# Feeding the feed-forward stage early: the first chunk's load waits for fewer scatters, and the last weight split moves into the last pair's second job

## The chip, the cores and the metric

The program runs on one core of a Trainium2 chip. The metric is the device time of one execution in microseconds. Engines are named as in the profile: PE (TensorE matmul), PEld (its weight load), DVE (VectorE), ACT (ScalarE), POOL (GpSimd) and SP (SyncE, which here only issues DMAs).

## The reference

Three layers run one behind the other over 4 x 576 = 2304 tokens of width 512, in float32.

```python
# attention: 4 batches, 8 heads, head_dim 64, causal window 128, slope bias, softmax
x = attn_out.transpose(0, 2, 1, 3).reshape(B * S, H * D)            # 2304 x 512
# mixture of experts, 8 experts of 512 -> 1024 -> 512
do_compute = x @ w_skip > 0;  xc = x[do_compute]
logits = xc @ w_gate;  e_idx = argmax(logits);  gate_w = softmax(logits)[e_idx]
for e in range(8):
    h = maximum(xc[e_idx == e] @ w1[e], 0)
    y[e_idx == e] = gate_w * (h @ w2[e])
x[do_compute] = xc + y
# feed-forward 512 -> 2048 -> 512
h = x @ w_in
g = h * tanh(log1p(exp(h)))
out = g @ w_out
```

With the inputs given, 1015 of the 2304 tokens go to an expert. Their counts by expert are 102, 111, 174, 146, 175, 133, 94, 80. Among the first 448 tokens they are 14, 17, 35, 24, 22, 45, 13, 9.

## The kernel before, in words

**Three stages in one program.** `attention` writes x to a DRAM tensor `tokens`, with the gate logits on the side. `experts` sorts the tokens by expert on the chip and corrects their rows in `tokens`. `feed_forward` reads `tokens` chunk by chunk and writes `out`. Every engine runs its own instruction stream, and counters (semaphores) are the only order between them.

**Experts.** Two experts form a pair (p = 0 to 3), and a job is 64 tokens of each of the two, 128 rows. The number of jobs of a pair is counted on the chip, at L984 to L1001, from the counts by expert. It goes to `jobs_i` in SBUF, from where each engine loads it into a register (`jobs_of`, L743). With the counts above, the pairs have 2, 3, 3 and 2 jobs. `all_jobs` (L757) writes job 0 without a condition and the others inside an `If` each: four in a row, then a loop. A job on PE (L1134) is `hidden` twice (32 matmuls), `transpose_h` twice, `output` twice (32 matmuls). DVE does two `relu` and one `scale_y` (L1030), which adds the scaled result to the gathered rows in `y_sb`. POOL gathers the rows of later jobs with an indirect DMA, and scatters `y_sb` to `tokens` (L835); each scatter adds 16 to `y_scattered[p]` when it has landed.

**Weights of the feed-forward stage.** Each fp32 weight is held as a high and a low part (fp32r), and a product takes three matmuls: lo x hi, hi x lo, hi x hi. `w_ffn` is 16 pieces of 1024 columns. Pieces 0 to 13 (`EARLY` = 14) are loaded during attention. ACT makes their high parts (`high_parts`, L902): 0 to 6 ahead of the last pair, 7 to 13 in its job 0. DVE makes the low parts (`low_parts`, L1022): 0 to 5 and 6 and 7 in job 0 of the last pair, 8 to 13 behind its last job (L1057). Pieces 14 and 15 land where the gathered rows `x_in` lie, so they are loaded after the experts, and are split in eight minis of 256 columns during chunk 0 (`SPLIT`, L1186). PE needs the early parts at the first `output`, and the minis at hidden block 12's `output` (L1432).

**Feed-forward.** Six chunks of 384 tokens. The x of a chunk is transposed by PE, and split by ACT (`xt_hi`) and DVE (`xt_lo`). A chunk has 16 steps f. In step f PE runs `hidden(f)`, 12 matmuls of 384 columns, and then `output(f - 3)`, 9 matmuls of 512 columns. Between the two, ACT and DVE work out g of block f: min, exp, a product, ln, exp, products, then `g_hi` and `g_lo`. In steps 3, 6, 9 and 12 (`AHEAD`) PE also transposes a quarter of the next chunk's x. SP issues, in this order: once all scatters of the last pair have landed, three loads of 128 tokens each for chunk 0 (L1278), the two last weight pieces (L1280), then the load of chunk 1 (L1266).

PE ends the experts with 20 dummy matmuls (`keep_warm`, L1156), then waits for the three loads and transposes them tile by tile (L1458).

## Time and profile before

| | |
|---|---|
| Median of 3 runs | 766.01 us (764.3 to 769.79) |
| Profiled execution, its own time | 767.03 us |
| Span in the profile | 765.2 us, mean granted clock 0.991 |
| PE busy | 742.9 us, 97% |
| DVE, ACT, POOL busy | 508.9, 366.6, 107.4 us |
| Experts' last matmul ends | 331.02 us |
| First matmul of the feed-forward proper | 343.97 us |

The span is the profile's own clock, from the first to the last instruction, and the execution's own time is 1.8 us longer. Attention fills the first 150 us, the experts 150 to 331 us, the feed-forward the rest. "Idle before" an instruction names who released it; "issue" there means that the profile shows no releaser. In a table by windows, the column PEclk is TensorE's granted clock, where 1.00 is 2.4 GHz and 0.50 is 1.2 GHz.

### The profile page before, as it was taken

How to read it: one execution, taken by the hardware profiler on the slowest of the kernel's cores; microseconds unless marked ns; L12 is line 12 of the kernel's file. 1: busy time of each engine (PE TensorE's matmuls, PEld its weight loads, DVE VectorE, ACT ScalarE, POOL GpSimd, SP SyncE). 2: the span in 40 equal slices, each digit the busy share in tenths (PEclk: the TensorE clock that was granted, in tenths of full speed). 3: DMA queues.
4: the chain of work that ended last, by engine and by line, in shares of the span. 5: the costliest groups of instructions: out<-in, count | busy, mean ns of one | idle time of the engine just before them, and what ended most of it. 6: DMA issues, size and time to landing. Idle time of an engine off the chain costs nothing.

```text
span 765.2 us, 13541 instructions
## 1 busy us (share of the span) xinstructions
PE 742.9 (97%) x4492; PEld 567.5 (74%) x4492; DVE 508.9 (67%) x1278; ACT 366.6 (48%) x887; POOL 107.4 (14%) x250
## 2 busy tenths in 40 slices
PE   7999999989999999989999999999999999999998
PEld 4887878773333333358989898998988989898986
DVE  4777777641111111647998888888788888888885
ACT  6888888301010103514655554555465545455544
POOL 4656655111110110000000000000000000000000
PEclk9999999989999999999999999999999999999999
DMA  8889988218782660031010101100110101001001
GB/s 300 250 261 279 277 265 234 65 39 327 281 310 87 257 248 23 15 104 41 1 43 1 42 0 42 38 5 2 42 41 0 41 0 41 0 0 42 1 0 42
DMA packets 53244, 78.23 MB, mean 102 GB/s; under 512 B 24739, under 2 KB 26403, under 8 KB 53152
## 3 DMA queue, kind: packets, MB, share of 16 engines
q1 hardware_dynamic: 51136, 72.02, 28.7%
q0 software_dynamic: 1600, 4.85, 1.7%
q8 instruction: 40, 0.66, 0.4%
q10 hardware_dynamic: 432, 0.41, 0.2%
q14 instruction: 36, 0.29, 0.1%
HBM read 65.53 MB, written 12.56 MB: 102 GB/s over the span
## 4 chain that ended last, share of the span: by engine, by line
PE 89%; DVE 5%; issue 2%; DMA 2%; ACT 1%; ACTq 0%; SPq 0%; DVEq 0%; POOLq 0%; POOL 0%
PE ps_y L1438 16%; PE ps_xt L1421 13%; PE ps_ht L1421 12%; PE ps_y L1128 9%; PE ps_h L1110 9%; PE ps_h L1438 8%; PE ps_out_t L586 5%; PE ps_probs_t L569 4%; PE ps_scores L558 4%; PE ps_x L597 4%; DVE h_sb L1020 1%; PE ps_ht L1117 1%; PE ps_h L1407 1%; PE ps_y L88 1%; DMA k_raw<-in_kT 1%
## 5 line engine op out<-in xcount | busy, mean ns | idle before, releaser
L1310 ACT ACTIVATE u_sb<-u_sb 128x384 f32<-128x384 f32 x96 | 50.6, 527 | 107.1 <-DVE u_sb L1358 107.1
L1314 ACT ACTIVATE r_sb<-n_sb,all_consts 128x384 f32<-128x384 f32 x96 | 59.3, 617 | 85.3 <-DVE n_sb L1374 85.3
L390 ACT ACTIVATE probs<-probs,neg_max 128x256 f32<-128x256 f32 (+2 forms) x160 | 72.6, 455 | 14.2 <-DVE neg_max L450 13.9
L1438 PE MATMUL ps_y<-ffn_lo,g_hi 128*128 128x512 f32 x192 | 76.6, 399 | 0.0
L1438 PE MATMUL ps_y<-ffn_hi,g_lo 128*128 128x512 f32 x192 | 75.9, 395 | 0.0
L1438 PE MATMUL ps_y<-ffn_hi,g_hi 128*128 128x512 f32 x192 | 75.7, 395 | 0.0
L1421 PE MATMUL ps_xt<-xt_hi,ffn_lo 128*128 128x384 f32 x192 | 66.9, 348 | 0.8 <-DVE xt_lo L1349 0.8
L1386 DVE SCALAR_TENSOR_TENSOR u_sb<-n_sb,r_sb 128x384 f32<-128x384 f32 x96 | 53.7, 559 | 19.1 <-ACT r_sb L1316 19.1
L1421 PE MATMUL ps_ht<-xt_hi,ffn_lo 128*128 128x384 f32 x192 | 66.0, 344 | 0.0
L1421 PE MATMUL ps_xt<-xt_hi,ffn_hi 128*128 128x384 f32 x192 | 65.5, 341 | 0.0
L1421 PE MATMUL ps_xt<-xt_lo,ffn_hi 128*128 128x384 f32 x192 | 65.4, 341 | 0.0
L1421 PE MATMUL ps_ht<-xt_hi,ffn_hi 128*128 128x384 f32 x192 | 64.9, 338 | 0.0
L1421 PE MATMUL ps_ht<-xt_lo,ffn_hi 128*128 128x384 f32 x192 | 64.8, 338 | 0.0
L1040 DVE SCALAR_TENSOR_TENSOR y_sb<-ps_y,x_in 128x512 f32<-128x512 f32 x10 | 7.5, 751 | 77.0 <-PE ps_y L1128 77.0
L450 DVE CUSTOM_DVE_ANT_0 probs<-ps_scores,bias_sb 128x256 f32<-128x256 f32 (+2 forms) x160 | 49.8, 362 | 8.8 <-PE ps_scores L558 8.6
L1363 DVE TENSOR_TENSOR g_lo<-n_sb,g_hi 128x384 fp32r<-128x384 f32 x96 | 52.6, 548 | 2.6 <-ACT g_hi L1329 2.6
L1020 DVE TENSOR_SCALAR h_sb<-ps_h 128x512 f32<-128x512 f32 x20 | 13.8, 691 | 60.6 <-PE ps_h L1110 60.6
L1374 DVE SCALAR_TENSOR_TENSOR n_sb<-u_sb 128x384 f32<-128x384 f32 x96 | 52.8, 550 | 0.7 <-ACT u_sb L1310 0.6
L1379 DVE TENSOR_TENSOR n_sb<-n_sb,r_sb 128x384 f32<-128x384 f32 x96 | 52.8, 550 | 0.0
L1368 DVE SCALAR_TENSOR_TENSOR r_sb<-u_sb,r_sb 128x384 f32<-128x384 f32 x96 | 52.8, 550 | 0.0
L1316 ACT ACTIVATE r_sb<-r_sb 128x384 f32<-128x384 f32 x96 | 50.4, 525 | 3.0
L919 ACT ACTIVATE h_t<-ps_ht 128x512 f32<-128x512 f32 x10 | 6.0, 598 | 93.5 <-PE ps_ht L1117 93.5
(174 smaller groups left out, 1628.4 us busy)
## 6 DMA issues: line engine op xcount, KB each, us to landing
w_sb<-in_w SPq DMA_DIRECT2D x8, 2048.0 KB, 11.9
ffn_raw<-in_w_ffn SPq DMA_DIRECT2D x16, 512.0 KB, 5.1
experts_even<-in_w SPq DMA_DIRECT2D x16, 512.0 KB, 5.8
experts_even<-in_w SPq DMA_DIRECT2D x4, 2048.0 KB, 12.7
q_raw<-in_qT SPq DMA_DIRECT2D x15, 288.0 KB, 4.1
k_raw<-in_kT SPq DMA_DIRECT2D x15, 288.0 KB, 4.9
v_sb<-in_v SPq DMA_DIRECT2D x16, 256.0 KB, 2.6
tokens<-x_out SPq DMA_DIRECT2D x64, 64.0 KB, 3.9
```

What stands on the lines that cost most here:

```text
L390: nc.scalar.activation(probs[0:n, r, h, 0:w], probs[0:n, r, h, 0:w], ACT.Exp, bias=neg_max[0:n, r, h:h + 1], scale=-1.0, accum_out=sums[0: ...
L1110: m = t_.matmul(ps_h[c][mine, :], x[:, k, mine], weights(p, 0, side, k * F1 + c * half), start=(k == 0), stop=(k == KD - 1))
L1128: m = t_.matmul(ps_y[slot][mine, :], (h_t, h_t2)[c][:, k, mine], weights(p, 1, side, (KD * c + k) * D), start=(c == 0 and k == 0), stop=(c ...
L1310: nc.scalar.activation(u_sb[:, t.r], u_sb[:, t.r], ACT.Exp).then_inc(u_ready, 1)
L1314: nc.scalar.activation(r_sb[:, t.r], n_sb[:, t.f % NB], ACT.Ln, bias=cst["two"]).then_inc(ln_ready, 1)
L1363: v.tensor_tensor(g_lo[:, t2.r], n_sb[:, t2.f % NB], g_hi[:, t2.r].bitcast(F32), ALU.subtract).then_inc(g_lo_ready, 1)
L1368: v.scalar_tensor_tensor(out=r, in0=u, scalar=2.0, in1=r, op0=ALU.subtract, op1=ALU.mult).then_inc(b_ready, 1)
L1374: v.scalar_tensor_tensor(out=n_sb[:, t.f % NB], in0=u_sb[:, t.r], scalar=2.0, in1=u_sb[:, t.r], op0=ALU.add, op1=ALU.mult).then_inc(n_read ...
L1379: v.tensor_tensor(n, n, r, ALU.mult).then_inc(ratio_ready, 1)
L1386: v.scalar_tensor_tensor(out=u, in0=n, scalar=2.0, in1=r, op0=ALU.add, op1=ALU.mult).then_inc(a_ready, 1)
L1421: m = nc.tensor.matmul(ps_h[t.f % HB][:, 0:C], ffn[a][:, at:at + P], b[:, t.par, k], start=(n == 0), stop=(n == 3 * KD - 1))
L1438: m = nc.tensor.matmul(ps_o[i][:, :], a[:, t.r, P * i:P * i + P], ffn[b][:, at:at + D], start=(t.f == 0 and n == 0), stop=(t.f == FT - 1 a ...
```

## The change

The first chunk's load waits for only those scatters of the last pair that can hold its tokens. The job count is taken a second time over the first 4 tiles (448 tokens, the chunk has 384), from the same running counts, with one matmul that takes both columns. `jobs_i` now holds 4 early counts, 4 counts of all, and 3 first-job numbers. The last pair has at least two jobs (`SURE` = 2, an empty one where there are fewer), written without a condition. The three tiles go to buffers that are free by then (`x_first` and two slots of `x_in`). PE transposes them quarter by quarter, and the 20 dummy matmuls are gone. DVE's low parts 8 to 13 move ahead of `scale_y` in job 1 of the last pair. SP issues the last two weight pieces once `scale_y` of the last job and PE's transposes are done, and chunk 1's load behind them once all scatters have landed. The minis move to steps 4, 5, 7, 8, 10, 11 and 13 (two of them). The PSUM banks of the feed-forward are dealt out anew, and PE gets a wait on the last `scale_y`, against a count loaded into a register, ahead of the first `output`.

```diff
-    ps_count = ps_h[0][:, 0:E]
+    ps_count = ps_h[0][:, 0:2 * E]
...
+    def early_jobs_of(eng, p):
+        return eng.value_load(jobs_i[0:1, p:p + 1], min_val=1, max_val=PHASE)
...
-    def all_jobs(eng, total, one):
+    def all_jobs(eng, total, one, sure=1):
...
-        one(0, 0)
-        rest(1)
+        for i in range(sure):
+            one(i, i % 2)
+        rest(sure)
...
-        then(v.tensor_scalar(jobs, jobs, 1.0, None, ALU.max))
+        then(v.tensor_tensor(early_and_all, early_and_all, cst["least"], ALU.max))
...
-            split = p == PH - 1 and isinstance(i, int) and i == 0
+            split = p == PH - 1 and isinstance(i, int) and i < SURE
             relu(p, i, 0)
             relu(p, i, 1)
             if split:
-                low_parts(range(0, 6))
+                low_parts(range(8, EARLY) if i else range(0, 6))
             scale_y(p, i, slot, before)
-            if split:
+            if split and not i:
                 low_parts(range(6, 8))
...
-        low_parts(range(8, EARLY))
...
-        t_.matmul(ps_count, ones, upto_tile[:, TT - 1], start=True, stop=True)
+        t_.matmul(ps_count, ones, upto_tile[:, EARLY_TILES - 1:TT:TT - EARLY_TILES], start=True, stop=True)
...
-        keep_warm(nc, ps_h[0], cst, 20)
...
-    SPLIT = {f: n for n, f in enumerate((1, 2, 4, 5, 7, 8, 10, 11))}
+    SPLIT = {4: (0,), 5: (1,), 7: (2,), 8: (3,), 10: (4,), 11: (5,), 13: (6, 7)}
...
-    ps_h, ps_xt, ps_o = banks[0:HB], banks[HB], banks[HB + 1:]
+    ps_h, ps_xt, ps_o = banks[2:HB] + banks[0:2], banks[HB], banks[HB + 1:]
-    first_xt = ps_o + [ps_xt]
+    first_xt = [ps_xt, ps_o[0]] + ps_h[2:HB]
+    x_early = own["x_early"]
...
-        sp.wait_ge(own["y_scattered"], own["jobs_of"](sp, PH - 1) * 16)
+        sp.wait_ge(own["y_scattered"], own["early_jobs_of"](sp, PH - 1) * 16)
         settled(sp, cst)
         for i in range(CT):
-            sp.dma_start(x_sb[:, i], dram["x"][P * i:P * i + P]).then_inc(tile_loaded[i], 16)
+            sp.dma_start(x_early[i], dram["x"][P * i:P * i + P]).then_inc(tile_loaded[i], 16)
+        total = own["jobs_of"](sp, PH - 1)
+        sp.wait_ge(own["y_scaled"], total)
+        settled(sp, cst)
+        sp.wait_ge(xt_ready, KD)
         for n in range(EARLY, PAIRS):
             sp.dma_start(ffn["raw"][:, n * 1024:n * 1024 + 1024], dram["w_ffn"][n]).then_inc(cst["w_loaded"], 16)
-        sp.wait_ge(xt_ready, KD)
+        sp.wait_ge(own["y_scattered"], total * 16)
+        settled(sp, cst)
         load(1)
...
             if isinstance(t.s, int) and t.s == 0:
                 pe.wait_ge(cst["w_lo_ready"], EARLY)
+                pe.wait_ge(own["y_scaled"], own["jobs_of"](pe, PH - 1))
...
         for i in range(CT):
             pe.wait_ge(tile_loaded[i], 16)
-            for k in range(KD):
-                m = nc.tensor.transpose(first_xt[k][:, P * i:P * i + P], x_sb[:, i, P * k:P * k + P], ident)
-                if i == CT - 1:
-                    m.then_inc(xt_ready, 1)
+        for k in range(KD):
+            for i in range(CT):
+                m = nc.tensor.transpose(first_xt[k][:, P * i:P * i + P], x_early[i][:, P * k:P * k + P], ident)
+            m.then_inc(xt_ready, 1)
```

How the instructions now stand, at three places. PE from the branch behind the last pair's jobs to the first matmul of the feed-forward (L88 is `keep_warm`, L1458 the transposes, L1421 `hidden`); before:

```order
L761 UNCONDITIONAL_BRANCH
L88 MATMUL ps_h<-all_consts 128x216 x20
L1400 UNCONDITIONAL_BRANCH
L1458 MATMUL ps_h<-all_consts,x_sb 128x128
L1458 MATMUL ps_y<-all_consts,x_sb 128x128 x2
L1458 MATMUL ps_h<-all_consts,x_sb 128x128 x2
...
L1421 MATMUL ps_xt<-xt_hi,ffn_lo 128x384
```

With the change (L1477 the transposes, L1438 `hidden`):

```order
L768 UNCONDITIONAL_BRANCH
L1477 MATMUL ps_h<-all_consts,x_first 128x128
L1477 MATMUL ps_h<-all_consts,x_in 128x128 x2
...
L1477 MATMUL ps_xt<-all_consts,x_first 128x128
L1477 MATMUL ps_xt<-all_consts,x_in 128x128 x2
...
L1438 MATMUL ps_ht<-xt_hi,ffn_lo 128x384
```

The dummy matmuls and a branch are gone, and the transposes come in groups of three, one group for each quarter of the width.

PE around the first `output` (L1456), behind `hidden(3)`, with the change; the register load and what belongs to it are new there:

```order
L1438 MATMUL ps_xt<-xt_hi,ffn_hi 128x384
L748 TENSOR_LOAD jobs_i
L748 ISA x2
L1456 MATMUL ps_h<-ffn_hi,g_lo 128x512
L1456 MATMUL ps_h<-ffn_lo,g_hi 128x512
```

The load stands behind the waits for `g_hi` and `g_lo` of block 0, so it begins when these are met.

DVE in the last pair, jobs 0 and 1 (`relu`, low parts, `scale_y`); before, and with the change:

```order
L1020 TENSOR_SCALAR h_sb<-ps_h 128x512 x2
L1027 TENSOR_TENSOR ffn_lo<-ffn_raw,ffn_hi 128x1024 x6
L1035 REGISTER_ALU
L1040 SCALAR_TENSOR_TENSOR y_sb<-ps_y,x_in 128x512
L1027 TENSOR_TENSOR ffn_lo<-ffn_raw,ffn_hi 128x1024 x2
L761 COMPARE_AND_BRANCH
L1020 TENSOR_SCALAR h_sb<-ps_h 128x512 x2
L1040 SCALAR_TENSOR_TENSOR y_sb<-ps_y,x_in 128x512
```

```order
L1029 TENSOR_SCALAR h_sb<-ps_h 128x512 x2
L1036 TENSOR_TENSOR ffn_lo<-ffn_raw,ffn_hi 128x1024 x6
L1044 REGISTER_ALU
L1049 SCALAR_TENSOR_TENSOR y_sb<-ps_y,x_in 128x512
L1036 TENSOR_TENSOR ffn_lo<-ffn_raw,ffn_hi 128x1024 x2
L1029 TENSOR_SCALAR h_sb<-ps_h 128x512 x2
L1036 TENSOR_TENSOR ffn_lo<-ffn_raw,ffn_hi 128x1024 x6
L1049 SCALAR_TENSOR_TENSOR y_sb<-ps_y,x_in 128x512
```

The branch between the two jobs is gone, and six low parts stand ahead of the second `scale_y`.

## Rows read from the trace of the kernel before

**Rows 1.** The page: busy time by engine, and the chain's shares by engine.

```profile
PE 742.9 (97%) x4492; PEld 567.5 (74%) x4492; DVE 508.9 (67%) x1278; ACT 366.6 (48%) x887; POOL 107.4 (14%) x250
...
PE 89%; DVE 5%; issue 2%; DMA 2%; ACT 1%; ACTq 0%; SPq 0%; DVEq 0%; POOLq 0%; POOL 0%
```

**Rows 2.** The chain that ended last, 324 to 409 us: start, length, what.

```profile
323.97 7.04 PE ps_y L1128 x32
...
331.04 0.76 DVE y_sb L1040
...
332.68 4.35 DMA tokens<-y_sb,scatter_list
...
337.99 4.44 DMA x_sb<-tokens
...
342.47 0.34 PE ps_h L1458
...
343.97 3.92 PE ps_xt L1421 x12
...
355.88 0.94 PE ps_h L1438 x3
...
406.02 2.12 PE ps_ht L1421 x12
408.14 0.70 PE ps_h L1438 x3
```

**Rows 3.** Timeline of POOL: start, length, instruction, idle before and releaser.

```profile
317.44 1.09 POOL L835 DMA_INDIRECT tokens<-y_sb,scatter_list  x1 [13.21 <-DVE y_sb L1040]
321.46 0.18 POOL L827 COPY scatter_list<-job_entry 128x1 int32<-128x1 int32 x1 [2.94 <-DMA tokens<-y_sb,scatter_list]
```

**Rows 4.** DMA issues, 300 to 366 us: KB each, median us to landing.

```profile
ffn_raw<-in_w_ffn SPq DMA_DIRECT2D x2, 512.0 KB, 5.7
x_sb<-tokens SPq DMA_DIRECT2D x1, 768.0 KB, 4.5
```

**Rows 5.** Timeline of DVE, the last pair's second job, and low parts behind it.

```profile
322.57 0.69 DVE L1020 TENSOR_SCALAR h_sb<-ps_h 128x512 f32<-128x512 f32 x1 [2.74 <-PE ps_h L1110]
...
331.71 6.89 DVE L1027 TENSOR_TENSOR ffn_lo<-ffn_raw,ffn_hi 128x1024 fp32r<-128x1024 f32 x6
```

**Rows 6.** Timeline of ACT, high parts 7 to 13.

```profile
312.60 6.72 ACT L905 ACTIVATE ffn_hi<-ffn_raw 128x1024 fp32r<-128x1024 f32 x7
```

**Rows 7.** Timeline of PE: the first tiles' transposes, and idle times before later matmuls.

```profile
342.47 0.33 PE L1458 MATMUL ps_h<-all_consts,x_sb 128*128 128x128 f32 x1 [1.31 <-DMA x_sb<-tokens]
342.64 0.38 PE L1458 MATMUL ps_y<-all_consts,x_sb 128*128 128x128 f32 x2
...
355.88 0.47 PE L1438 MATMUL ps_h<-ffn_hi,g_lo 128*128 128x512 f32 x1 [1.65 <-issue]
```

**Rows 8.** Windows: length, busy time of PE, PEld, DVE, ACT, POOL, PEclk, DMA.

```profile
160.00:162.00 2.00, 2.00 (x11) 2.00 (x11) 2.00 (x7) 0.00 (x0) 0.00 (x0) 0.50 0.00 0
...
346.00:347.00 1.00, 1.00 (x4) 1.00 (x4) 0.00 (x0) 0.00 (x0) 0.00 (x0) 0.50 1.02 395
```

**Rows 9.** Timeline of PE, PE idle times at 159 and 203 us.

```profile
159.18 4.27 PE L1074 MATMUL ps_h<-what,at_row 128*128 128x40 f32 x20 [2.32 <-DVE at_row L1011]
...
203.54 1.94 PE L1110 MATMUL ps_h<-w_sb,x_first 128*64 128x512 f32 x8 [1.24 <-issue]
```

**Rows 10.** Timelines of SP and of POOL, 171 to 175 us.

```profile
171.01 15.36 SPq L782 DMA_DIRECT2D w_sb<-in_w  x4
...
174.80 0.18 POOL L811 COPY job_entry<-table 128x1 int32 x1 [6.57 <-issue]
```

**Rows 11.** Timeline of DVE, chunk 0, last instruction of step 14.

```profile
407.15 0.56 DVE L1386 SCALAR_TENSOR_TENSOR u_sb<-n_sb,r_sb 128x384 f32<-128x384 f32 x1 [0.19 <-ACT r_sb L1316]
```

**Rows 12.** Timeline of DVE: a mini, and a wait for issue.

```profile
358.43 0.42 DVE L1393 TENSOR_TENSOR ffn_lo<-ffn_raw,ffn_hi 128x256 fp32r<-128x256 f32 x1
...
552.63 0.56 DVE L1358 TENSOR_SCALAR u_sb<-ps_xt 128x384 f32<-128x384 f32 x1 [2.83 <-issue]
```

More of the change, by code:

```diff
@@ L57 @@
 JOBS = PHASE + PH
+SURE = 2
+EARLY_TILES = 4
 LOG_W = W.bit_length() - 1
@@ L678, in experts @@
     by_pair = scratch(PH * PH).rearrange("p (a b) -> p a b", a=PH)
-    chunks = scratch(E).rearrange("p (a b) -> p a b", a=PH)
-    jobs, ends, first1 = (scratch(PH) for _ in range(3))
+    chunks = scratch(2 * E).rearrange("p (a b) -> p a b", a=2 * PH)
+    early_and_all, ends, first1 = scratch(2 * PH), scratch(PH), scratch(PH)
+    jobs = early_and_all[:, PH:2 * PH]
     tables = ffn["tables"]
@@ L684, in experts @@
     assert used[0] <= SCRATCH, used[0]
-    count_i = sb("count_i", [P, E], I32)
-    jobs_i = sb("jobs_i", [1, 2 * PH], I32)
+    count_i = sb("count_i", [P, 2 * E], I32)
+    jobs_i = sb("jobs_i", [1, 3 * PH], I32)
     table = sb("table", [P, JOBS + PHASE + 12], I32)
@@ L936, in _ @@
                 high_parts(range(7))
-            all_jobs(act, totals[p], functools.partial(one, p, total=totals[p], split=(p == PH - 1)))
+            all_jobs(act, totals[p], functools.partial(one, p, total=totals[p], split=(p == PH - 1)),
+                     SURE if p == PH - 1 else 1)
     @block.vector
@@ L987, in _ @@
         v.tensor_copy(rank_i, rank)
-        then(v.tensor_copy(chunks, count_i[:].rearrange("p (a b) -> p a b", a=PH)))
+        then(v.tensor_copy(chunks, count_i[:].rearrange("p (a b) -> p a b", a=2 * PH)))
         v.tensor_scalar(row_i, rank_i, W - 1, None, ALU.bitwise_and)
         v.tensor_scalar(chunk_i, rank_i, LOG_W, None, ALU.logical_shift_right)
-        then(v.tensor_reduce(jobs, chunks, AX_X, ALU.max))
+        then(v.tensor_reduce(early_and_all, chunks, AX_X, ALU.max))
         v.tensor_copy(row, row_i)
         v.tensor_copy(rank, chunk_i)
-        then(v.tensor_scalar(jobs, jobs, 1.0, None, ALU.max))
+        then(v.tensor_tensor(early_and_all, early_and_all, cst["least"], ALU.max))
         v.tensor_tensor(row, row, side, ALU.add)
@@ L998, in _ @@
         then(v.tensor_reduce(ends, by_pair, AX_X, ALU.add))
-        v.tensor_copy(jobs_i[:, 0:PH], jobs[0:1, :])
+        v.tensor_copy(jobs_i[:, 0:2 * PH], early_and_all[0:1, :])
         then(v.scalar_tensor_tensor(out=first1, in0=ends, scalar=1.0, in1=jobs, op0=ALU.add, op1=ALU.subtract))
-        v.tensor_scalar(jobs_i[:, PH:2 * PH], first1[0:1, :], -1.0, None, ALU.add).then_inc(jobs_ready, 1)
+        v.tensor_scalar(jobs_i[:, 2 * PH:3 * PH], first1[0:1, :], -1.0, None, ALU.add).then_inc(jobs_ready, 1)
         then(v.tensor_tensor(work.rearrange("p t (a b) -> p t a b", a=PH), by_expert.rearrange("p (a b t) -> p t a b", a=PH, b=2),
@@ L1055, in _ @@
         for p in range(PH):
-            all_jobs(dve, totals[p], functools.partial(one, p, before=totals[p - 1] if p else None))
-        low_parts(range(8, EARLY))
+            all_jobs(dve, totals[p], functools.partial(one, p, before=totals[p - 1] if p else None),
+                     SURE if p == PH - 1 else 1)
     @block.tensor
@@ L1332, in step @@
                 xt_part(*ahead, AHEAD[f])
-            if isinstance(c, int) and c == 0 and f in SPLIT:
-                piece = mini(SPLIT[f])
+            for n in SPLIT.get(f, ()) if isinstance(c, int) and c == 0 else ():
+                piece = mini(n)
                 act.wait_ge(cst["w_loaded"], 16 * PAIRS)
@@ L1389, in step @@
                 xt_part(*ahead, AHEAD[f - 1])
-            if isinstance(c, int) and c == 0 and f - 1 in SPLIT:
-                piece = mini(SPLIT[f - 1])
-                dve.wait_ge(cst["w_hi_ready"], EARLY + SPLIT[f - 1] + 1)
+            for n in SPLIT.get(f - 1, ()) if isinstance(c, int) and c == 0 else ():
+                piece = mini(n)
+                dve.wait_ge(cst["w_hi_ready"], EARLY + n + 1)
                 v.tensor_tensor(ffn["lo"][:, piece], ffn["raw"][:, piece], ffn["hi"][:, piece].bitcast(F32),
@@ L1456, in _ @@
             pe.wait_ge(tile_loaded[i], 16)
-            for k in range(KD):
-                m = nc.tensor.transpose(first_xt[k][:, P * i:P * i + P], x_sb[:, i, P * k:P * k + P], ident)
-                if i == CT - 1:
-                    m.then_inc(xt_ready, 1)
+        for k in range(KD):
+            for i in range(CT):
+                m = nc.tensor.transpose(first_xt[k][:, P * i:P * i + P], x_early[i][:, P * k:P * k + P], ident)
+            m.then_inc(xt_ready, 1)
         run_steps(pe, step, LAG)
-CONSTS = {"ident": P, "two": 1, "index_m8": E, "odd": E, "upto": PH * PH, "job1": JOBS, "token": TT, "empty": 1}
+CONSTS = {"ident": P, "two": 1, "index_m8": E, "odd": E, "upto": PH * PH, "job1": JOBS, "token": TT, "empty": 1,
+          "least": 2 * PH}
 TABLES = {"not_before": P, "ones": P, "rows": P, "same_expert": E * TT}
@@ L1524, in shape_constants @@
         "two": np.full((P, 1), 2.0),
+        "least": np.tile([1.0] * (2 * PH - 1) + [SURE], (P, 1)),
     }
```

10 lines of the change are left out of this document (7 added, 3 removed).

## The prediction

> **What bounds the kernel now.** I read the page first: PE is busy for 742.9 of 765.2 us and holds 89% of the chain that ended last [rows 1]. So only time in which PE stands still, does dummy work or runs at the lower clock can be won. The chain of waits around the change says where that is. The last matmul of the experts ends at 323.97 + 7.04 = 331.01 us, and the first of the feed-forward starts at 343.97 us [rows 2]. In those 12.96 us the chain goes through `scale_y` on DVE, the last scatter (it lands at 332.68 + 4.35 = 337.03), the load of x (337.99 + 4.44 = 342.43), a transpose and two splits [rows 2]. PE's 20 dummy matmuls in there do nothing for the result. Then the first hidden block takes 3.92 us, where the same twelve matmuls later take 2.12 [rows 2]; the table by windows gives the reason, a granted clock of 0.50, which is 1.2 GHz, against 1.00 at other times [rows 8]. Last, the first `output` starts at 355.88, 7.99 us after the first hidden block is done (343.97 + 3.92 = 347.89): that is the fill of the DVE and ACT pipeline [rows 2]. PE has run ahead by then and idles 1.65 us before it [rows 7]. From there on the chain is PE alone, so whatever moves the first `output` moves the end.
>
> **Part by part.** All the times below are on the profile's clock.
>
> *The early load.* With the routing of these inputs the first 448 tokens give the last pair 13 and 9 tokens, one job; the early count is 1 of 2. Job 0's scatter, issued at 317.44, has landed when POOL copies its next list at 321.46 [rows 3]. Before, it took 342.43 - 337.03 = 5.40 us from a landed scatter to landed tiles [rows 2]; so now they land by 321.46 + 5.40 = 326.9, 4.1 us ahead of the end of the last job. The load is hidden, and so is the last scatter. If that cover went, each us beyond 4.1 would cost one.
>
> *PE from the last job to the first hidden block.* Transposes can start at 331.01. Before, 1.50 us passed from the last tile's first transpose (342.47 [rows 7]) to the first matmul at 343.97 [rows 2]. Now a quarter is whole after three transposes, not after one; consecutive ones start 0.17 us apart [rows 7], so 2 x 0.17 = 0.34 is added. The first matmul starts at 331.01 + 1.50 + 0.34 = 332.85. That is **11.12 us earlier**. `scale_y` stands ahead of the first `xt_lo` on DVE, but runs from 331.04 for 0.76 us [rows 2], so until 331.80, and the first `xt_lo` has only to be done by 332.85. It costs nothing.
>
> *The clock.* PE no longer has 5 us of mostly idle time ahead of hidden block 0. It should run at 2.4 GHz, in 2.12 us to the next block's start, and with the last matmul's tail (a 128x384 matmul's record is longer than its pitch by about 0.17) in 2.29 to its result, instead of 3.92: **1.63 us**. Result at 335.14.
>
> *Low parts 8 to 13.* Six take 6.89 us [rows 5]. They start when the second `relu` ends, 322.57 + 0.69 = 323.26, and end at 330.15; `scale_y` is not due before 331.04. Their high parts are done at 312.60 + 6.72 = 319.32 [rows 6]. Cost nothing, with 0.9 us of cover; each us beyond it delays `scale_y` and then `xt_lo`.
>
> *The register load.* The wait for the last `scale_y` is met long before. But its count is loaded into a register, behind the waits for `g_hi` and `g_lo`, with PE idle. The trace has no such load on PE in the open. The nearest rows: POOL signals before 171.01, where SP's DMAs start on that signal, and then loads six such registers before its copy at 174.80 [rows 10]. That is 3.79 / 6 = 0.63 us each at most, and in other places they are hidden (0). I take 0.63, since nothing runs beside it here. Bounds 0 and 1.3 (twice, if PE's is slower). **+0.63**. The Trainium skill speaks of about 600 ns as the floor of a tensor load (DMA: Bandwidth & Descriptors, Latency and other measured facts), and elsewhere of about 200 ns a register (Runtime: NRT & Kernel Launch, Instruction fetch mechanics); by the second the sum would be 0.4 us better.
>
> *The first output.* 335.14 + 7.99 + 0.63 = 343.76, against 355.88: 12.12 us earlier.
>
> *The minis.* Weights 14 and 15 are issued at about 333, 5.4 us earlier than before, and take 5.7 us to land [rows 4]; the first mini is at step 4, after 343.8. DVE gets two at step 14, and PE needs them for block 12's `output` in step 15. Before, the last DVE instruction of step 14 ends at 407.15 + 0.56 = 407.71 [rows 11] and that `output` starts at 408.14 [rows 2]. Two minis of 0.42 [rows 12] end by 408.55 at most, 0.4 late; instructions on DVE overlap a little, so I take **+0.3**. Bounds 0 (DVE ahead, since steps 2 and 3 lose their minis) and 0.8.
>
> *Chunk 1's load.* It moves behind the two weight pieces and the last scatter. In the worst case the scatter waits until both pieces have landed, at 333.0 + 0.9 + 5.7 = 339.6; then 0.4 to issue and 4.5 to land [rows 4] makes 344.5. PE's transposes for it come behind the first `output`, nine matmuls at 0.70 / 3 each [rows 2], so at 343.76 + 2.1 = 345.9. Hidden, by 1.4 us at the worst.
>
> *Router and SP.* Twice as many columns in six instructions of 0.2 us, and one register load more on SP, which waits anyway: nothing.
>
> *Sum.* -11.12 - 1.63 + 0.63 + 0.3 = **-11.82 us**. Against the profiled execution's own 767.03 us that makes 755.2. It lies 1.0 us above the median of 766.01, so against the median I forecast **754.2 us**. With a free register load and free minis the sum would be -12.75, or 753.3.
>
> **Rivals.**
>
> *A. The clock falls before the first output.* PE's hole there grows: hidden block 3 ends at 332.85 + 4 x 2.12 + 0.17 = 341.5, and the output starts at 343.76, so 2.26 us of idle, against 1.65 [rows 7]. For it: an idle time of 2.32 us at 159.18 [rows 9] was followed by a granted clock of 0.50 [rows 8]. Against it: the 1.65 us were not, and PE is busy without a break for 8 us ahead. Price: the stretch at 1.2 GHz that began at 344 us cost the 1.63 us worked out above. The one at 160 us may have been longer: a mean clock of 0.991 leaves room for 2 x 0.009 x 765 = 14 us at 1.2 GHz in all. I take once to twice 1.63. Time 755.8 to 757.5.
>
> *B. A taken branch is no longer covered.* The first instructions behind the last pair come by a branch over two jobs and a loop. After the first pair, also of two jobs, PE stood still for 1.24 us at such a branch [rows 9], with no engine to wait for; DVE once for 2.83 [rows 12]. Against it: at this very place PE went on into the dummy matmuls without a hole, and there is one branch fewer. Price 1.2 to 2.8 less DVE's and ACT's slack of 0.4: 755.2 to 757. The Trainium skill says that a taken branch to a target outside the two fetched pages stalls the engine until it is fetched (Runtime: NRT & Kernel Launch, Instruction fetch mechanics); the row at 203.54 agrees, and the one at 331 does not, so the rule alone decides nothing here.
>
> *C. The change does not do what it says.* If the early count came out as 2, the tiles would land near 342.4 as before, at best 1.5 us sooner for want of the weights beside them, PE would idle for 10 us and start at 1.2 GHz, and the register load and the minis add 0.9: 765.5 to 767. Against it is the count of 13 and 9.
>
> *D. Slower.* The clock falls in the hole as in A, and stays at 1.2 GHz, since PE then waits step by step on nothing that would raise it. Every us of PE's full-clock work costs one more, so from 11.8 us of such work, a stretch of 24 us at the lower clock, the kernel is slower than before; through the 13 steps left of chunk 0 (4.2 us each) it would be 754 + 55 = 809. Against it: all such stretches in this trace together have at most 14 us.
>
> **How the numbers follow.** The forecast case 0.62 (its own range 752.5 to 755.5), A 0.17, B 0.12, C 0.03, D 0.02, and 0.04 for something unseen, half of it between -1% and +1%. A difference of 1%, 7.7 us, is about what a measurement here can tell from none; 766.01 less that is 758.35. The forecast, A and B lie below it, C above. Faster 0.93, same 0.05, slower 0.02. For the range the lower end is the sum without register load and minis (753.3) and 1.7 us for how far a median of this kernel may move (runs shown lie 1.7 below and 3.8 above it); the upper end takes in A and B, and 0.7 of that: 751.6 to 758.2.
>
> **What would show it.** Right: PE's first transposes of the feed-forward follow the last job's matmul within 0.3 us and no wait for a DMA; twelve matmuls of hidden block 0 in 2.1 us at clock 1.00; six low parts between `relu` and the second `scale_y`, with DVE still waiting for PE; the first `output` 0.6 us later after `g_lo` than before; PE idle about 0.3 us ahead of step 15's output. Wrong: a granted clock of 0.50 behind the first output (A), idle ahead of the transposes with "issue" (B), tiles landing behind 331 (C), or PE waiting for chunk 1's load in step 3.

## The result, and the profile after

The changed kernel takes 756.17 us (median of 4 runs, 753.83 to 757.14) against 767.04 us for the kernel before on the same chip (4 runs, 764.3 to 769.79). The medians are 10.9 us apart. The ratio, which is estimated from all these runs and is not the quotient of the medians (0.9858), is 0.9842, with a 95% interval of 0.9816 to 0.9869: 12.1 us less, between 10.0 and 14.1. The forecast was 754.2 us (751.6 to 758.2). The profiled execution took 753.83 us by its own time, with a span of 752.0 us at a mean granted clock of 0.991, the clock of the profile before.

The page of the changed kernel, where [rows 1] stood before, says that the bound is the same: PE lost 9.5 us of work (40 matmuls fewer: each of the 20 dummies shows as two) and 3.7 us of idle time, and the DMA's share of the chain is 1% instead of 2%, by the page's rounding.

```profile
PE 733.4 (98%) x4452; PEld 559.9 (74%) x4452; DVE 509.6 (68%) x1278; ACT 366.7 (49%) x887; POOL 107.2 (14%) x250
...
PE 89%; DVE 5%; issue 2%; ACT 2%; DMA 1%; POOL 0%; SPq 0%; DVEq 0%; ACTq 0%; POOLq 0%
```

The chain that ended last, in the same place as [rows 2] (start, length, what):

```profile
322.94 7.02 PE ps_y L1137 x32
329.96 0.49 PE ps_h L1477 x3
330.47 0.50 ACT xt_hi L1321
330.99 0.57 DVE xt_lo L1366
331.61 2.40 PE ps_ht L1438 x12
...
340.79 1.86 issue
342.64 0.96 PE ps_h L1456 x3
343.60 2.12 PE ps_y L1456 x6
345.72 0.64 PE ps_h L1424 x3
346.36 2.65 PE ps_ht L1438 x12
...
395.76 0.77 DVE ffn_lo L1410 x2
...
396.67 0.94 PE ps_h L1456 x3
```

The experts' last matmul ends at 322.94 + 7.02 = 329.96, and the transposes of the feed-forward follow at once. No DMA is left in this part of the chain. Hidden block 0 starts at 331.61 and takes 2.40 us, not 3.92. The first `output` starts at 342.64. Then there is something that the fixed sum did not have: six `output` matmuls in 2.12 us (later 1.41) and a hidden block in 2.65 (later 2.11). The windows of PE (columns as in [rows 8]) tell why.

```profile
342.00:344.00 2.00, 1.36 (x6) 1.14 (x7) 1.85 (x4) 1.11 (x3) 0.00 (x0) 1.00 0.00 0
344.00:346.00 2.00, 2.00 (x8) 1.50 (x7) 1.93 (x5) 0.97 (x3) 0.00 (x0) 0.51 0.00 0
346.00:348.00 2.00, 2.00 (x10) 2.00 (x9) 1.78 (x5) 1.44 (x3) 0.00 (x0) 0.64 0.00 0
```

The clock fell to 1.2 GHz at 344.0 us, for 3.4 us, behind an idle time of PE (a hole) of 2.31 us. PE has a second, smaller hole 54 us later, ahead of block 12's `output`; the clock did not fall there (timeline of PE; idle time before and its releaser stand in brackets, as in [rows 7]):

```profile
342.64 0.50 PE L1456 MATMUL ps_h<-ffn_hi,g_lo 128*128 128x512 f32 x1 [2.31 <-issue]
...
396.67 0.47 PE L1456 MATMUL ps_h<-ffn_hi,g_lo 128*128 128x512 f32 x1 [0.41 <-DVE ffn_lo L1410]
```

The early load itself, in the timelines of SP and of POOL. The last scatter is issued at 331.64, and at 321.25 SP already loads:

```profile
321.25 0.34 SPq L1290 DMA_DIRECT2D x_first<-tokens  x1
...
331.45 0.81 SPq L1296 DMA_DIRECT2D ffn_raw<-in_w_ffn  x2
...
331.64 0.98 POOL L843 DMA_INDIRECT tokens<-y_sb,scatter_list  x1 [10.14 <-DVE y_sb L1049]
...
336.73 0.38 SPq L1278 DMA_DIRECT2D x_sb<-tokens  x1
```

So the early count did come out as 1. A load of these tiles takes about 3.1 us to land by the profile's table of DMA issues, so they are there at about 325, 5 us ahead of PE. Chunk 1's load is issued at 336.73 and takes 4.4 us: it is there at 341.1, and PE's first transpose for it starts at 345.72.

**Where the gain comes from.** Each profile can be cut at two matmuls: E, the end of the experts' last, and O, the start of the first `output`. From E to O it was 24.89 us and is now 12.69: 12.20 less. From O to the end it was 409.35 and is 409.39. Of the span's 13.2 us the remaining 1.0 lies ahead of E, where every execution differs (the last section). The second part is level only because gains and losses in it cancel. The table has the distances between successive `output` starts; a step is the time from one to the next.

| us | before | after | difference |
|---|---|---|---|
| E to O | 24.89 | 12.69 | -12.20 |
| step 1 behind O | 4.64 | 6.21 | +1.57 |
| step 12 (the two minis) | 4.23 | 4.78 | +0.55 |
| an ordinary step, median | 4.227 | 4.207 | -0.02 |
| all of O to end but steps 1, 12 and 48 | 395.26 | 393.38 | -1.88 |
| step 48, at a branch of the chunk loop | 5.23 | 5.02 | -0.21 |
| O to end | 409.35 | 409.39 | +0.04 |

**The 24.89 us are those of one execution.** The kernel before has two near twins among the experiments: one has its PSUM banks in another order, the other eight unused columns of constants. Their profiles take 20.66 and 23.61 us from E to O. The chain of the first, to be laid beside [rows 2]:

```profile
337.11 2.50 DMA tokens<-y_sb,scatter_list
...
340.57 3.58 DMA x_sb<-tokens
...
345.70 2.40 PE ps_ht L1421 x12
```

The last scatter takes 2.50 us there and not 4.35, the load 3.58 and not 4.44, and hidden block 0 runs at 2.4 GHz, in 2.40 us and not 3.92. That is the whole difference of 4.23 us. The changed kernel takes 12.67 to 12.69 us from E to O in each of the four profiles in which PE's work up to O is the same. So the change takes 8.0 to 12.2 us out of this stretch, depending on the execution that it is laid beside, and the profile behind [rows 2] is at the upper end. The timed runs spread in the same way: those of the kernel before lie between 762.0 and 771.3 us in all sets together, those of the changed one between 753.8 and 757.4. From O to the end it is the other way round: 409.39 us is the changed kernel's longer case, and 407.92 a repeat of it (next section).

### The profile page after: what moved, and what is told of

It is laid out like the page before. It is cut to its first block, busy times and chain, and to the rows that moved or that the text cites. A ratio compares the mean times of both kernels' runs of the same rounds, so it can differ in the third digit from the quotient of the medians.

```text
span 752.0 us, 13468 instructions
## 1 busy us (share of the span) xinstructions
PE 733.4 (98%) x4452; PEld 559.9 (74%) x4452; DVE 509.6 (68%) x1278; ACT 366.7 (49%) x887; POOL 107.2 (14%) x250
## 4 chain that ended last, share of the span: by engine, by line
PE 89%; DVE 5%; issue 2%; ACT 2%; DMA 1%; POOL 0%; SPq 0%; DVEq 0%; ACTq 0%; POOLq 0%
PE ps_y L1456 16%; PE ps_ht L1438 13%; PE ps_xt L1438 12%; PE ps_y L1137 9%; PE ps_h L1119 9%; PE ps_h L1456 8%; PE ps_out_t L588 5%; PE ps_probs_t L571 4%; PE ps_scores L560 4%; PE ps_x L599 4%; DVE h_sb L1029 1%; PE ps_h L1424 1%; PE ps_ht L1126 1%; PE ps_y L90 1%; DMA k_raw<-in_kT 1%
## 5 line engine op out<-in xcount | busy, mean ns | idle before, releaser
L1456 PE MATMUL ps_y<-ffn_hi,g_lo 128*128 128x512 f32 x192 | 76.5, 399 | 0.0
L1456 PE MATMUL ps_y<-ffn_hi,g_hi 128*128 128x512 f32 x192 | 76.5, 398 | 0.0
L1456 PE MATMUL ps_y<-ffn_lo,g_hi 128*128 128x512 f32 x192 | 75.9, 395 | 0.0
L1438 PE MATMUL ps_ht<-xt_hi,ffn_lo 128*128 128x384 f32 x192 | 66.2, 345 | 0.2 <-DVE xt_lo L1366 0.2
L1438 PE MATMUL ps_xt<-xt_hi,ffn_lo 128*128 128x384 f32 x192 | 65.7, 342 | 0.0
L1438 PE MATMUL ps_ht<-xt_lo,ffn_hi 128*128 128x384 f32 x192 | 65.2, 339 | 0.0
L1438 PE MATMUL ps_ht<-xt_hi,ffn_hi 128*128 128x384 f32 x192 | 65.1, 339 | 0.0
L1438 PE MATMUL ps_xt<-xt_lo,ffn_hi 128*128 128x384 f32 x192 | 65.0, 339 | 0.0
L1438 PE MATMUL ps_xt<-xt_hi,ffn_hi 128*128 128x384 f32 x192 | 64.9, 338 | 0.0
```

Source lines behind the costliest of these rows:

```text
L1438: m = nc.tensor.matmul(ps_h[t.f % HB][:, 0:C], ffn[a][:, at:at + P], b[:, t.par, k], start=(n == 0), stop=(n == 3 * KD - 1))
L1456: m = nc.tensor.matmul(ps_o[i][:, :], a[:, t.r, P * i:P * i + P], ffn[b][:, at:at + D], start=(t.f == 0 and n == 0), stop=(t.f == FT - 1 a ...
```

## Experiments: why the clock fell

Two theories stood against each other. The first: the hole in PE's work ahead of the first `output` grew from 1.65 to 2.31 us, and that brings the clock down for a stretch, which costs 1.5 us. The rival: the stretch is a matter of chance or comes with the phase of the whole program, and the hole has no part in it. A third question was whether the register load, the minis and the dropped dummies are worth what the prediction said. All edits are against the changed kernel unless another is named. In each result the ratio is to the kernel before, run in the same set.

**The changed kernel once more**, unedited.

> The changed kernel itself, beside the others of this set. By theory 1 the clock falls behind the first output in this profile too (hole of 2.3 us), step 1 takes 6.2 us, step 12 4.8, and the ratio to before is 0.984 to 0.986. By the rival (the clock falls by chance of where the hole lies) it may stay at 1.00 here, with step 1 at 4.6 us and a kernel 1.6 us faster in that execution.

Measured: 756.48 us (755.02 to 757.36, 6 runs), ratio 0.9864 (0.9837 to 0.9892). Its profile has the same hole in PE's timeline, and by the windows no fall:

```profile
345.29 0.50 PE L1456 MATMUL ps_h<-ffn_hi,g_lo 128*128 128x512 f32 x1 [2.31 <-issue]
```

```profile
344.00:346.00 2.00, 0.71 (x3) 0.62 (x4) 1.97 (x6) 1.01 (x2) 0.00 (x0) 1.00 0.00 0
346.00:348.00 2.00, 2.00 (x13) 1.64 (x12) 1.82 (x4) 1.29 (x4) 0.00 (x0) 1.00 0.00 0
```

Step 1 took 4.64 us here, and O to the end 407.92. The first theory's expectation, a fall here too, failed. So the fall is not fixed to the kernel: the same hole brought it in one profile and not in the other. Was the hole needed at all? The next runs vary it.

**The register load ahead of the transposes**, so that the hole is back at its old size.

```
-                pe.wait_ge(own["y_scaled"], own["jobs_of"](pe, PH - 1))
+                pe.wait_ge(own["y_scaled"], last_total)
...
+        last_total = own["jobs_of"](pe, PH - 1)    # ahead of the first transposes
```

> PE loads the count into a register ahead of its first transposes, not ahead of the first output. Theory 1 (the load costs PE 0.65 us in the open, and the hole it makes, 2.31 us instead of about 1.67, is what lets the clock fall to 1.2 GHz): the first output starts 8.0 us after hidden block 0 is done, not 8.63, the granted clock stays 1.00 behind it, and the kernel is 2.2 us faster than the changed one (0.65 for the load, 1.57 for the clock), some 14.4 us faster than before. Rival (the clock falls by chance of where the hole lies, whatever its length): 0.65 us faster only, the clock falls in this profile too.

Measured: 755.29 us (754.66 to 756.21), ratio 0.9863 (0.9837 to 0.9889). The chain:

```profile
335.58 2.38 PE ps_ht L1438 x12
...
345.95 0.93 PE ps_h L1456 x3
```

From hidden block 0 to the first `output` it is 345.95 - 335.58 = 10.37 us, against 342.64 - 331.61 = 11.03: the load in the open is worth 0.66 us. Ahead of the transposes it costs 0.17 (block 0 at E + 1.82 instead of E + 1.65), so 0.50 is won. The hole is 1.66 us and the clock did not fall. The time does not show the gain: 14.4 us less than before was expected, the ratio gives 10.5 (8.5 to 12.5), no better than the unedited kernel's 0.9842 and 0.9864. What is said of this edit rests on its profile.

**Five dummy matmuls in the hole.**

```
+            if isinstance(c, int) and c == 0 and f == LAG:
+                keep_warm(nc, ps_o[0], cst, 5)     # between hidden(3) and the first output
```

> Five dummy matmuls of 216 columns (about 0.19 us a record, two records each, so 1.9 us) run on PE between hidden block 3 and the first output; the register load stays where the change put it. Theory 1 (idle time lets the clock fall): the clock stays 1.00 behind the first output, step 1 takes 4.6 us instead of 6.2, and the kernel is 1.6 us faster than the changed one, 13.7 faster than before. Rival (the clock falls for another reason, such as the load of the first outputs themselves): no gain, or the dummies' end delays the first output by up to 0.3 us.

Measured: 754.82 us (752.62 to 755.44), ratio 0.9852 (0.9825 to 0.9879). The chain:

```profile
343.09 1.82 PE ps_h L90 x10
...
345.41 0.95 PE ps_h L1456 x3
```

The hole shrinks to 0.49 us, and the output stands where it was, at E + 12.69: the dummies cost nothing. Step 1 took 4.63 us, no fall. The expected 1.6 us beyond the changed kernel are too few for these intervals to show or to rule out.

**The hole made longer**: the first `output` waits for one `g_hi` more.

```
-            pe.wait_ge(g_hi_ready, t.s + 1)
+            pe.wait_ge(g_hi_ready, 2 if isinstance(t.s, int) and t.s == 0 else t.s + 1)
```

> The changed kernel, in which the first output also waits for the high part of block 1's g. PE idles about 4.9 us there instead of 2.3. It costs 2.6 us by itself. Theory 1, as left by the repeated profile (a hole of 2.3 us lets the clock fall in some executions and not in others; a longer one in all): the clock falls in this profile, step 1 takes 6.2 us or more, and the kernel is 2.6 + 1.6 to 3.3 us slower than one whose clock did not fall, 759 to 762. Rival (the length of the hole does not matter): 2.6 us slower, clock 1.00.

Measured: 760.36 us (757.95 to 768.72, 10 runs), ratio 0.9915 (0.9886 to 0.9945). The timeline of PE, and the windows around it:

```profile
348.19 0.79 PE L1456 MATMUL ps_h<-ffn_hi,g_lo 128*128 128x512 f32 x1 [4.83 <-ACT g_hi L1346]
```

```profile
346.00:348.00 2.00, 0.00 (x0) 0.00 (x0) 1.78 (x4) 1.48 (x3) 0.00 (x0) 0.64 0.00 0
348.00:350.00 2.00, 1.80 (x4) 1.49 (x5) 2.00 (x5) 0.93 (x2) 0.00 (x0) 0.50 0.00 0
350.00:352.00 2.00, 2.00 (x6) 1.54 (x5) 1.14 (x3) 0.73 (x2) 0.00 (x0) 0.50 0.00 0
```

The output comes 2.5 us later. The clock is at 0.50 for 6.8 us, twice as long as in the changed kernel's profile and from 1.7 us ahead of the output on, and step 1 takes 7.00 us. One of the ten runs, the one of 768.72 us, has a mean clock of 0.933, where the others have 0.984 to 0.989; no profile of it exists, and what held it up is not known.

**Dummy matmuls behind the last job**, where the change dropped them.

```
+        keep_warm(nc, ps_h[0], cst, 20)            # behind PE's jobs
```

> The changed kernel with the 20 dummy matmuls back between the last pair and the transposes. Theory (they are dead weight once x is there): 7.5 us of PE time ahead of the transposes, the first hidden matmul 9.2 us behind the end of the experts instead of 1.65, and 7.5 us slower than the changed kernel, about 764. Rival (they cover the last weight pieces or the fill of ACT and DVE, so that part comes back): 3 to 6 us slower.

Measured: 764.19 us (762.8 to 765.06), ratio 0.9956 (0.9937 to 0.9975). The chain:

```profile
325.94 7.02 PE ps_y L1137 x32
332.95 7.50 PE ps_h L90 x40
...
341.95 2.38 PE ps_ht L1439 x12
```

Block 0 starts at E + 9.00, 7.35 us later than without them, and by the ratios to the kernel before the program is 7 to 9 us slower than the changed one. The clock had nothing to gain there: block 0 takes 2.4 us with and without. And though PE is busy from 332.95 on for 17.7 us, with no gap over 0.2 us, the hole of 2.32 us ahead of the first `output` was followed by a fall at 353.2 and a step 1 of 6.19 us. The prediction had held 8 busy us ahead of the hole against rival A; here twice as much did not prevent the fall.

Together, over the profiles of all kernels here: with a hole of 0.2 to 1.7 us (seven kernels) the clock never fell behind it; with 2.3 to 2.4 us it fell in four of six profiles; with 4.83 us it fell, for twice as long. The timed runs can be read by their mean clock, if less surely: 3.4 us at half the clock are 0.5 x 3.4 / 752 = 0.0023 of it. A short or a long stretch at the start of the program (the last section) and the one near 160 us alone make 0.993 or 0.989, which the profiles without a fall show (0.988 to 0.993); a fall of 3.4 us more makes 0.991 or 0.986. In the kernels with the hole of 2.3 to 2.4 us and without the dummies behind the last job (the changed one and its repeat, the minis one to a step, the one with 64 bytes more; the last two below) 14 of 21 runs stand at 0.991 or 0.986. In the three with a short hole (the early register load, the five dummies, and the three edits at once, below) it is 1 of 18.

At this place the longer hole is needed, and at 2.3 us it is not enough every time. The first theory holds, but not in its form "always"; the rival, with the hole having no part in it, falls. The length of the hole is not all that counts, though. Near 160 us, ahead of the matmuls of [rows 9], PE has a hole of 2.32 to 2.35 us in all 14 profiles, behind 4 us of dummy matmuls, and there the clock fell in all 14, each time for 6.8 us. What differs between the two places was not tested.

## Experiments: the other steps

**The full count for the early load** (rival C built on purpose).

```
-        sp.wait_ge(own["y_scattered"], own["early_jobs_of"](sp, PH - 1) * 16)
+        sp.wait_ge(own["y_scattered"], own["jobs_of"](sp, PH - 1) * 16)
```

> The first load waits for all scatters of the last pair again; all else as changed. Theory (the early load is what takes scatter and load off the path): tiles land at about 342 on the clock of the kernel before, PE idles some 10 us and starts at 1.2 GHz, and the kernel is within 2 us of before, 11 to 13 us slower than the changed one. Rival (the gain came from the moved low parts and the dropped dummies, the load being hidden anyway): no more than 3 us slower than the changed one.

Measured: 766.68 us (764.93 to 768.38, 10 runs), ratio 1.0004 (0.9978 to 1.0029). Its chain has the DMAs back:

```profile
334.68 2.36 DMA tokens<-y_sb,scatter_list
...
338.00 3.34 DMA x_in<-tokens
...
344.27 3.35 PE ps_ht L1438 x12
```

All else of the change is kept, and nothing is won that the time shows. Without SP's shorter wait the whole gain is gone.

**Low parts 8 to 13 behind the last job again.**

```
-            if split:
-                low_parts(range(8, EARLY) if i else range(0, 6))
+            if split and not i:
+                low_parts(range(0, 6))
...
+        low_parts(range(8, EARLY))
```

> DVE's low parts 8 to 13 go back behind the second scale_y; all else as changed. Theory: they take 6.89 us between scale_y (ends at 330.75) and the first xt_lo, so hidden block 0 starts about 6.7 us later, at 338.3, and the kernel is 6 to 8 us slower than the changed one (more if PE's hole of 6.7 us also lowers the clock: up to 1.7). Rival (the first output waits for them, but not hidden block 0, as the weight's low parts are only wanted there): 0 to 1 us slower.

Measured: 764.06 us (761.47 to 766.62), ratio 0.9972 (0.9949 to 0.9994). The timeline of DVE:

```profile
333.94 0.75 DVE L1049 SCALAR_TENSOR_TENSOR y_sb<-ps_y,x_in 128x512 f32<-128x512 f32 x1 [7.78 <-PE ps_y L1138]
334.61 6.89 DVE L1036 TENSOR_TENSOR ffn_lo<-ffn_raw,ffn_hi 128x1024 fp32r<-128x1024 f32 x6
```

The 6.89 us now stand between `scale_y` and the first `xt_lo`. Block 0 starts at E + 8.13, 6.48 us later, and at the lower clock, since PE idles ahead of it: the first `output` is 8.3 us later. The move of the low parts is therefore worth nothing by itself (the run before this one) and 8 us once the load is early: the gain needs both edits. In the changed kernel they stand where DVE waited for PE anyway, and 0.97 us of that wait is left:

```profile
321.54 0.69 DVE L1029 TENSOR_SCALAR h_sb<-ps_h 128x512 f32<-128x512 f32 x1 [2.74 <-PE ps_h L1119]
322.14 6.89 DVE L1036 TENSOR_TENSOR ffn_lo<-ffn_raw,ffn_hi 128x1024 fp32r<-128x1024 f32 x6
...
330.00 0.75 DVE L1049 SCALAR_TENSOR_TENSOR y_sb<-ps_y,x_in 128x512 f32<-128x512 f32 x1 [0.97 <-PE ps_y L1137]
```

**Minis one to a step, in steps 1, 2, 4, 5, 7, 8, 10 and 11.**

```
-    SPLIT = {4: (0,), 5: (1,), 7: (2,), 8: (3,), 10: (4,), 11: (5,), 13: (6, 7)}
+    SPLIT = {f: (n,) for n, f in enumerate((1, 2, 4, 5, 7, 8, 10, 11))}
```

> The eight minis go back to steps 1, 2, 4, 5, 7, 8, 10 and 11, one each; all else as changed. Theory (two minis in step 14 of DVE make PE wait at block 12's output, and nothing else of their move matters, since the weights have landed by 337): step 12 takes 4.21 us instead of 4.78, 0.55 us faster than the changed kernel. Rival (the early minis take DVE and ACT time in the fill, or wait for the weights): as fast as the changed kernel or up to 1 us slower.

Measured: 755.28 us (754.6 to 757.33), ratio 0.9854 (0.9826 to 0.9882). In the profile step 12 takes 4.21 us instead of 4.78, so the two minis cost 0.57 us. The first `output` stands at E + 12.68 as without the edit, so the two minis in steps 1 and 2 delay nothing that PE waits for. The timed difference to the unedited kernel, 1.2 us, is within the intervals.

**Three edits at once**: early register load, four dummies in the hole, minis one to a step.

> Three edits on the changed kernel: the register load ahead of the first transposes, four dummy matmuls (1.5 us) ahead of the first output, and the minis as in the kernel before. Theory: the gains add, 0.5 for the load, 1.6 for the clock, 0.55 for the minis, 2.6 us faster than the changed kernel, about 753.5 where the changed one has 756. Rival (each recovers the same slack): no more than 1.8 us.

Measured: 753.90 us (753.67 to 754.83), ratio 0.9833 (0.9807 to 0.986), the lowest median of all. Its slowest run lies below the fastest of the unedited kernel in the same set (755.02); between the medians are 2.6 us. The timeline of PE:

```profile
342.97 1.62 PE L90 MATMUL ps_h<-all_consts 128*128 128x216 f32 x8
344.80 0.47 PE L1456 MATMUL ps_h<-ffn_hi,g_lo 128*128 128x512 f32 x1 [0.20 <-issue]
```

By the profiles 1.43 us of this are fixed (E to the end 419.18 against 420.61): 0.66 by the first `output`, 0.57 by step 12, 0.2 in small pieces. Block 0 starts at E + 1.65 here, so the 0.17 us that the register load seemed to cost ahead of the transposes did not come again. The fall that all but never comes here and its 1.5 us, in some runs of the other, fit the remainder; it is within what medians of this kernel move. Against the kernel before it is 14.2 us less by the medians, 12.8 (10.7 to 14.8) by the ratio.

## Experiments: the steps of 4.207 us

The changed kernel does each ordinary step 0.02 us faster, with the same matmuls. Two edits of the change could touch all of them: the PSUM banks dealt out anew, and eight columns more in the tile of constants, which move every SBUF tile placed behind it by 32 bytes. Each was tried alone, **in the kernel before**.

The banks:

```
-    ps_h, ps_xt, ps_o = banks[0:HB], banks[HB], banks[HB + 1:]
+    ps_h, ps_xt, ps_o = banks[2:HB] + banks[0:2], banks[HB], banks[HB + 1:]
```

> The kernel before with one line changed: the PSUM banks of the hidden blocks in the order that the change deals them out. The profile before has steps of 4.23 us, that of the changed kernel and of four variants 4.21, 1.9 us over the stage. Theory 2 (the pitch is a matter of the execution or the chip, not of the banks): no difference in time to before. Rival (the new deal of banks makes matmuls 0.4% faster): 1.5 to 2 us faster than before, ratio 0.998.

Measured: 766.58 us (763.83 to 769.66, 12 runs), ratio 0.9996 (0.9974 to 1.0019). Steps of 4.227 us, O to end 409.38. All steps but 1, 12 and 48 take 395.26 us together, as before. The order of the banks does nothing here.

The constants:

```
-CONSTS = { ... "token": TT, "empty": 1}
+CONSTS = { ... "token": TT, "empty": 1, "pad": 8}      # eight columns of zeros that nothing reads
```

> The kernel before with eight unused columns at the end of its table of constants, as the change adds eight ("least"). Everything placed in SBUF behind them, the split x and g among it, moves by 32 bytes. Theory 3 (where x and g lie in SBUF sets the pitch of the feed-forward's matmuls): a step takes 4.21 us as in the changed kernel, not 4.23, and the kernel is 1.9 us faster than before, ratio 0.9975. Rival (the pitch hangs on something else of the change): 4.23, no difference.

Measured: 765.65 us (762.1 to 767.28, 12 runs), ratio 0.996 (0.994 to 0.998). The chain of waits:

```profile
566.91 2.12 PE ps_xt L1421 x12
...
571.12 2.11 PE ps_xt L1421 x12
```

From one hidden block to the next it is 571.12 - 566.91 = 4.21 us. The same place in the kernel before:

```profile
570.67 2.12 PE ps_xt L1421 x12
...
574.90 2.12 PE ps_ht L1421 x12
```

There it is 4.23. The median step is 4.207 us, and all steps but 1, 12 and 48 take 393.40 us together instead of 395.26: 1.9 us from eight columns that hold nothing. From O to the end it is 407.23 instead of 409.35. The other 0.2 us are step 48, which takes 5.02 us here; they can't be put down to the columns, since kernels with the same constants show 5.02 to 5.34 (5.22 with the early register load, 5.34 with the minis one to a step). The timed gain by the ratio, 0.4% or 3 us (1.5 to 4.6), agrees.

And eight columns more **in the changed kernel**, 64 bytes in all:

```
-          "least": 2 * PH}
+          "least": 2 * PH, "pad": 8}
```

> The changed kernel with eight unused columns more, so that all behind the constants lies 64 bytes further than in the kernel before, and 32 further than in the changed one. Theory 3, if 64 bytes are as good as none: steps of 4.23 us, and 1.9 us slower than the changed kernel, about 758. Rival: 4.21 and no difference.

Measured: 756.87 us (median of 6 runs), ratio 0.9851 (0.9823 to 0.9879). One of the six took 906.58 us at a mean clock of 0.749; the ratio leaves it out, the median of the other five is 756.62, and what held it up is not known. The clock fell in step 1 (6.05 us). The median step, 4.216 us, misleads: the steps alternate between 4.18 and 4.22 us, and all but 1, 12 and 48 take 392.79 us together, 0.6 less than the 393.38 of the changed kernel. So neither expectation came true. The slow steps of the kernel before do not come back with 64 bytes, and this is the fastest of the three placements by its one profile. The sum tells them apart well: it is 395.26 in both profiles without the extra columns and 393.3 to 393.5 in all eleven with eight of them. No rule of the shift can be given from three placements.

## Why the prediction was right

**The first hidden block: right.** Forecast 11.12 us earlier, measured 12.98 - 1.65 = 11.33 relative to E. This is against the very execution that the forecast was worked out from; against the two twins of the kernel before it is 8.62 and 10.17. So the path was right, and that the size fits to 0.2 us says less than it seems to. The 0.34 us for a quarter that needs three transposes was the right kind of term; the transposes started at once.

**The clock in block 0: right.** 3.92 became 2.40 us; forecast was 1.63 less, measured 1.52. The granted clock is 1.00 there now. But in one twin of the kernel before, block 0 took 2.40 us already, so this term is there to be won in some executions only.

**The low parts: right.** They end 0.97 us ahead of `scale_y`'s release; 0.9 was forecast. The run with them behind the last job showed the price of that cover.

**The register load: right.** 0.64 us from the profile (8.63 us from block 0's result to the first `output`, 7.99 before), 0.66 when moved ahead of the transposes; 0.63 forecast, from a row on POOL. The Trainium skill's floor of about 600 ns for a tensor load (DMA: Bandwidth & Descriptors, Latency and other measured facts) agrees with this row; its 200 ns a register (Runtime: NRT & Kernel Launch, Instruction fetch mechanics) is not what the load costs in the open.

**The first output: right.** Forecast 12.12 us earlier, measured 12.20, with the same reserve: beside the twins it is 8.0 and 10.9.

**The minis: right mechanism, size off.** Forecast 0.3, measured 0.55 to 0.57. The two minis take 0.77 us in the chain, a little less than the 2 x 0.42 of the forecast. What the sum left out is the way from DVE's end to PE's start, 396.53 to 396.67, 0.14 us. PE's idle time of 0.41 us and the 0.17 by which a matmul's record is longer than its pitch make up the whole of the delay.

**Chunk 1's load: right**, with 4.6 us to spare, not 1.4: the worst case for the scatter did not come.

**Rival A: came true in part, and the fixed sum missed it.** It was given 0.17 and a price of 1.6 to 3.3 us. The price was right at its lower end (1.57), the chance too low: it came in four of the six profiles with this hole, and by the mean clocks in two thirds of the timed runs. What was wrong was to count PE's 8 busy us ahead of the hole as evidence against it. The evidence for it, the hole of 2.32 us at 159.18, was stronger than one row: at that place the hole brings the fall in all 14 profiles.

**Rival B: no.** Transposes follow the last job within 0.1 us. (Its times were added up wrongly: 1.2 to 2.8 less 0.4 on top of 754.2 makes 755.0 to 756.6, not 755.2 to 757.) The row:

```profile
329.89 0.33 PE L1477 MATMUL ps_h<-all_consts,x_first 128*128 128x128 f32 x1
```

The Trainium skill's rule on taken branches (Runtime: NRT & Kernel Launch, Instruction fetch mechanics) would have a stall wherever the target is not yet fetched; this row has none, so here either the fetch was covered or none was due. No run tells which.

**Rival C: not here**, and its price, 765.5 to 767, was met by the run built for it (766.68). **Rival D: no**; behind the hole of 2.3 us the clock came back after 3.4 us in each profile in which it fell, and after 6.8 us behind the longest hole. The runs of 768.72 and 906.58 us, of two edited kernels, had lower mean clocks (0.933 and 0.749) than stretches of this length make; without a profile it stays open whether theirs was such a case.

**What the sum did not have**: the 1.9 us from the placement of the constants. The prediction took it that only time in which PE stands still, does dummy work or runs at the lower clock can be won; the pitch of the matmuls can change too. These 1.9 us and the 0.2 of step 48 hid the fall of the clock and half of the minis. The forecast of -11.82 against -12.17 from E to the end is close because +1.57 and +0.25 more were paid, and 2.09 and 0.08 were given back. Without the shift the same kernel's median would be, by 756.17 + 1.88, about 758.1, just inside the range. And the 11.1 us of the first term are those of the slowest of three executions. The mechanism was right by its terms; the closeness of the total is partly luck.

**Open.** Why a shift by 32 bytes speeds up PE's steps by 0.5%, and why with 64 bytes they alternate. What decides, for a hole of 2.3 us, whether the clock falls, always near 160 us and in two of three cases ahead of the first `output`. Why the last scatter and the load take 6.1 us in one execution of the kernel before and 8.8 in another. And how much of the 1.0 us ahead of E is the change's: the router has changed too, but E moves by more than this from one execution to the next.

## What to carry to other kernels

Where a stage waits for a whole set of writes, ask which of them its first piece needs; if a count on the chip can tell, waiting for those alone takes the whole latency of write, issue and load off the path, but only if the other engines' preparations (here DVE's low parts) are moved out of the way in the same edit. After such a move look at the hole of PE that is next: it costs its own length, and here, at 2.3 us, a stretch at half the clock in four profiles of six. A few dummy matmuls that ended before the data came cost nothing, and no fall was seen with them. Profile the kernel before more than once: here the way through scatter, load and first block differed by 4 us between executions, and a forecast from one profile takes over its luck. Compare the steady steps of both kernels as well, by their sum and not by the median alone, since an added constant can move every tile and be worth as much as a term of the sum.
